# Block-diagonal full-array products and identities on VectorE in the inversion of a delta-rule attention

## The reference

```
k_n = k / (norm(k) + 1e-6);  state = zeros(B, H, 48, 48)
for t in range(768):
    y[t]  = q[t] @ state
    v_old = state^T k_n[t]
    state = state + beta[t] * outer(k_n[t], v[t] - v_old)
x = y as (3072, 384)
# experts: logits = x @ w_gate; e = argmax; out = gate * sigmoid(x @ w_output_gate)[e] * relu(x @ w1[e]) @ w2[e]
# last:    max(x @ w1, x @ w2, x @ w3) @ w_out
```

## Time and profile before

| | us |
|---|---|
| runs (median of 3) | 1111.56 (1108.06 to 1112.52) |
| the profiled execution's own time | 1108.98 |
| its span | 1107.3 |
| TensorE busy | 1026.3 |
| VectorE busy | 509.7 |
| ScalarE busy | 366.9 |
| GpSimd busy | 335.4 |

### The profile page before, as it was taken

The page is one execution under the profiler, slowest core; times in us unless marked ns, Lnnn a source line. Parts: engine busy times, 40 slices in busy tenths (PEclk is TensorE's granted clock), DMA queues, the critical chain, the costliest instruction groups (busy, mean ns, idle before and its releaser), DMA issues. The chain is left out here.

```text
span 1107.3 us, 30948 instructions
## 1 busy us (share of the span) xinstructions
PE 1026.3 (93%) x13260; PEld 895.4 (81%) x13260; DVE 509.7 (46%) x1085; ACT 366.9 (33%) x731; POOL 335.4 (30%) x251
## 2 busy tenths in 40 slices
PE   4898999999999999849999999999599999999998
PEld 3787888887888778737999999998488888888888
DVE  5575665666666655435444444433332323233221
ACT  1455544554555455412222222221121222122111
POOL 3444253435233422115352555525310001000000
PEclk9999998999999999958999999999699999999999
DMA  9212112121212111044344444223201010100000
GB/s 313 110 34 65 55 53 60 55 72 41 72 58 70 41 44 34 9 151 162 102 155 165 171 165 171 86 86 114 71 22 39 19 44 14 48 16 22 15 15 29
DMA packets 58056, 84.90 MB, mean 77 GB/s; under 512 B 28880, under 2 KB 52816, under 8 KB 55376
## 3 DMA queue, kind: packets, MB, share of 16 engines
q1 hardware_dynamic: 52272, 46.94, 13.5%
q0 software_dynamic: 5664, 36.18, 9.6%
HBM read 61.67 MB, written 21.43 MB: 75 GB/s over the span
## 5 line engine op out<-in xcount | busy, mean ns | idle before, releaser
L1081 PE MATMUL hb<-early,last_h 128*128 128x512 f32 x648 | 208.0, 402 | 1.2 <-DVE early L1213 1.2
L1081 PEld LDWEIGHTS hb<-early,last_h 128*128 128x128 f32 x648 | 121.7, 191 | 29.4 <-DVE early L1213 1.6
L1081 PE MATMUL hb<-early,last_l 128*128 128x512 f32 x324 | 129.3, 399 | 0.0
L1219 DVE TENSOR_TENSOR m<-hb,m 128x512 f32<-128x512 f32 x36 | 24.9, 692 | 132.3 <-PE hb L1081 132.3
L329 PEld LDWEIGHTS bank<-t,n_hi 64*64 64x64 f16 x2688 | 65.7, 111 | 23.6 <-issue 7.9
L540 DVE TENSOR_TENSOR p<-bank,cf 128x512 f16<-128x512 f32 x96 | 66.1, 689 | 32.2 <-PE bank L329 31.8
L329 PE MATMUL bank<-t,n_hi 64*64 64x64 f16 x2688 | 72.7, 195 | 4.9 <-issue 4.2
L1081 PE MATMUL ob<-wo_h,early 128*128 128x384 f32 x288 | 75.1, 339 | 0.0
L1081 PEld LDWEIGHTS hb<-early,last_l 128*128 128x128 f32 x324 | 61.6, 190 | 15.0
L1003 POOL TENSOR_TENSOR late<-w_raw,late 128x3072 fp32r<-128x3072 f32 x8 | 54.5, 6812 | 57.6 <-DVE late L943 57.3
L1114 POOL DMA_INDIRECT rows<-y_sorted,idx x24 | 23.0, 959 | 159.1 <-DVE scaled L1209 155.8
(11 more groups left out here) (163 smaller groups left out, 2194.7 us busy)
## 6 DMA issues: line engine op xcount, KB each, us to landing
w_raw<-w POOLq DMA_DIRECT2D x14, 1536.0 KB, 7.6
kq_t<-qh SPq DMA_DIRECT2D x24, 256.0 KB, 3.3
y_sorted<-y_sb SPq DMA_DIRECT2D x31, 192.0 KB, 1.9
x_in<-x_sorted SPq DMA_DIRECT2D x29, 192.0 KB, 2.8
k_raw<-kt_in SPq DMA_DIRECT2D x24, 192.0 KB, 3.2
v_in<-vh SPq DMA_DIRECT2D x24, 192.0 KB, 3.6
k_own<-kh SPq DMA_DIRECT2D x24, 192.0 KB, 3.4
out<-o_sb SPq DMA_DIRECT2D x24, 192.0 KB, 1.8
```

Source lines behind the costliest of these rows:

```text
L1081: ins = pe.matmul(out, a[x], b[y], start=first and i == 0, stop=last and i == 2, skip_group_check=True)
L1219: dve.tensor_tensor(m1[f % 2][:], h_bank[f % 2][1][:, :], m0[f % 2][:], ALU.max).then_inc(m1_out, 1)
```

## The change

In the inversion of the attention stage:
- The identities of the three jacobi rounds and of the residual are no longer added by PE. VectorE adds them when it reads PSUM: instead of a multiplication by the block mask it now does an addition of the identity, and in the residual (which moves from ScalarE to VectorE) of twice the identity.
- Since the mask is no longer applied to the result, N is masked beforehand: GpSimd computes n_base, N times the mask of 4x4 blocks, in slot 2, and jacobi waits for it in place of n_hi.
- "inv" is one product, residual plus twice the identity times the transpose, so that the product of t16 and the identity goes.
- Five groups (prod at four levels and N times t16 in the residual) use n_both: for each head a 128x128 block-diagonal matrix with both halves' N, so that 8 full-array matmuls with 64 columns take the place of 16. ScalarE fills n_both with two copies behind n_hi; its zeros are written once at the start. Minus t16 in the residual is one full-array matmul of 512 columns.
- Five parts of the norm move one slot ahead, GpSimd's kn waits for beta_k from the second step on, and in "lg" VectorE reads the logits from PSUM instead of waiting for its own copy.

```diff
-    ch[:, CH_REP:CH_REP + U * C] = np.tile(row == col, (1, U))
+    ch[:, CH_REP:CH_REP + C] = row == col
...
-    NORM = {1: [0], 2: [1], 3: [2, 10], 5: [3], 6: [4], 7: [5], 8: [6, 13], 9: [7, 8, 9], 14: [11], 15: [12]}
+    NORM = {1: [0], 2: [1], 3: [2, 10], 4: [3], 5: [4], 6: [5], 7: [6], 8: [7, 8, 9, 13], 14: [11], 15: [12]}
...
+        def both_heads(lhs, rhs, out, first=False):
+            for u in range(U):
+                ins = pe.matmul(out[:, C * u:C * u + C], lhs[:, u].rearrange("q h c -> q (h c)"), rhs(u), start=first and u == 0,
+                                stop=True, skip_group_check=True)
+            return ins
+        def whole(lhs, rhs, out, first):
+            return pe.matmul(out[:, :], lhs, rhs, start=first, stop=True, skip_group_check=True)
...
             elif what == "jacobi":
-                    pe.wait_ge(n_hi_ready[st], k + 1)
+                    pe.wait_ge(n_base_ready[st], k + 1)
...
-                diagonal(ident16, ident_rep, pb, True)
-                each_head(n, eye if lv == 0 else t, pb).then_inc(jacobi_done[st], 1)
+                each_head(nb, eye if lv == 0 else t, pb, first=True).then_inc(jacobi_done[st], 1)
...
             elif what == "prod":
...
-                each_head(n, t, pb, first=True).then_inc(prod_done[st], 1)
+                both_heads(n_both[st], lambda u: t16[st][:, u, :], pb, first=True).then_inc(prod_done[st], 1)
...
             elif what == "resid":
-                diagonal(ident16, ident_rep, pb, True)
-                diagonal(neg16, flat(t16[st]), pb, False)
-                each_head(n, t, pb)
+                whole(neg16, flat(t16[st]), pb, True)
+                both_heads(n_both[st], lambda u: t16[st][:, u, :], pb)
                 each_head(nl, t, pb).then_inc(resid_done[st], 1)
             elif what == "inv":
...
-                each_head(t, eye, ttb, first=True)
                 pe.wait_ge(resid_out[st], k + 1)
-                each_head(pr, tt, ttb).then_inc(inv_done[st], 1)
+                each_head(pr, tt, ttb, first=True).then_inc(inv_done[st], 1)
... (ScalarE)
                 act.copy(n_hi[st][:], n_kb_a[par][st][:, :, 0, :]).then_inc(n_hi_ready[st], 1)
+                for hh, s in enumerate(half):
+                    ins = act.copy(n_both[st][s, :, hh, :], n_kb_a[par][st][s, :, 0, :])
+                ins.then_inc(n_both_ready[st], 1)
...
-            elif what == "resid":
-                act.copy(p16[st][:], pb).then_inc(resid_out[st], 1)
... (VectorE)
-                dve.tensor_tensor(t16[st][:], pb, mask_of(None), ALU.mult).then_inc(jacobi_out[st], 1)
+                dve.tensor_tensor(t16[st][:], pb, of_heads(CF_EYE), ALU.add).then_inc(jacobi_out[st], 1)
+            elif what == "resid":
+                dve.wait_ge(resid_done[st], k + 1)
+                dve.tensor_tensor(p16[st][:], pb, of_heads(CF_TWO), ALU.add).then_inc(resid_out[st], 1)
...
-                dve.tensor_copy(logits[:, to, :], yb[st][:, X:X + 2 * E]).then_inc(logit_out[st], 1)
-                dve.wait_ge(logit_out[st], k + 1)
-                dve.tensor_reduce(best[:, st:st + 1], logits[:, to, 0:E], AX.X, ALU.max).then_inc(routed[st], 1)
+                dve.tensor_reduce(best[:, st:st + 1], yb[st][:, X:X + E], AX.X, ALU.max).then_inc(routed[st], 1)
+                dve.tensor_copy(logits[:, to, :], yb[st][:, X:X + 2 * E])
... (GpSimd)
             if what == "kn":
-                pool.wait_ge(inv_norm, k + 1)
+                if k >= 1:
+                    pool.wait_ge(beta_k_ready, k + 1)
+                else:
+                    pool.wait_ge(inv_norm, 1)
...
+            elif what == "split":
+                pool.wait_ge(gram_out[st], 2 * k + 2)
+                pool.tensor_tensor(n_base[st][:], n_kb_a[par][st][:, :, 0, :], of_heads(CF_BASE), ALU.mult).then_inc(n_base_ready[st], 1)
```

More of the change, by code:

```diff
@@ L40 @@
 CF_BASE = CF_LV + (LEVELS - 2) * C
-CF_IOTA = CF_BASE + C
+CF_EYE = CF_BASE + C
+CF_TWO = CF_EYE + C
+CF_IOTA = CF_TWO + C
 CF_STEP = CF_IOTA + E
@@ L49 @@
 CH_REP = CH_NEG + P
-CH_TRI = CH_REP + U * C
+CH_TRI = CH_REP + C
 CH_ONE = CH_TRI + P
@@ L69, in constants @@
         cf[:, CF_LV + (lv - 2) * C:CF_LV + (lv - 1) * C] = below & ((col >> lv) == (row >> lv) - 1)
-    cf[:, CF_BASE:CF_BASE + C] = (row >> 2 == col >> 2) & (row >= col)
+    cf[:, CF_BASE:CF_BASE + C] = row >> 2 == col >> 2
+    cf[:, CF_EYE:CF_EYE + C] = row == col
+    cf[:, CF_TWO:CF_TWO + C] = 2.0 * (row == col)
     cf[:, CF_IOTA:CF_IOTA + E] = E - np.arange(E)
@@ L129, in attention_and_router @@
     n_hi = single("n_hi", [P, U, C], F16)
+    n_both = single("n_both", [P, U, 2, C], F16)
     n_lo = single("n_lo", [P, U, C], F16)
+    n_base = single("n_base", [P, U, C], F16)
     t16 = single("t16", [P, U, C], F16)
@@ L177, in attention_and_router @@
     n_lo_ready = pair_of("n_lo_ready")
+    n_both_ready = pair_of("n_both_ready")
+    n_base_ready = pair_of("n_base_ready")
     kb_ready = pair_of("kb_ready")
@@ L217, in attention_and_router @@
     neg16 = ch[:, CH_NEG:CH_NEG + P]
-    ident_rep = ch[:, CH_REP:CH_REP + U * C]
+    eye16 = ch[:, CH_REP:CH_REP + C]
     tri16 = ch[:, CH_TRI:CH_TRI + P]
@@ L342, in eye @@
         def eye(s, u):
-            return ident_rep[s, 0:C]
+            return eye16[s, :]
         def inv(k, par, st, what, lv):
             tb, ttb, pb = bank[st]
-            n, nl, t, tt, pr = (lambda s, u, x=x[st]: x[s, u, :] for x in (n_hi, n_lo, t16, tt16, p16))
+            nl, nb, t, tt, pr = (lambda s, u, x=x[st]: x[s, u, :] for x in (n_lo, n_base, t16, tt16, p16))
             if what == "kt":
@@ L517, in norm, with clear @@
                 act.activation(nrm[:, 1], nrm[:, 0], ACT.Sqrt).then_inc(rooted, 1)
+                if k == 0:
+                    clear(n_both[1])
+        def clear(x):
+            for hh, s in enumerate(half):
+                act.copy(x[s, :, 1 - hh, :], zeros[s, 0:C].unsqueeze(1).broadcast_to((C, U, C)))
         act.wait_ge(zeros_ready, 1)
         act.activation(root_of_zero[:], zeros[:, 0:1], ACT.Sqrt)
+        clear(n_both[0])
         act.wait_ge(blank, 1)
@@ L561, in chain @@
                 to = 2 * k + st
-                dve.tensor_copy(logits[:, to, :], yb[st][:, X:X + 2 * E]).then_inc(logit_out[st], 1)
-                dve.wait_ge(logit_out[st], k + 1)
-                dve.tensor_reduce(best[:, st:st + 1], logits[:, to, 0:E], AX.X, ALU.max).then_inc(routed[st], 1)
+                dve.tensor_reduce(best[:, st:st + 1], yb[st][:, X:X + E], AX.X, ALU.max).then_inc(routed[st], 1)
+                dve.tensor_copy(logits[:, to, :], yb[st][:, X:X + 2 * E])
                 dve.wait_ge(routed[st], 5 * k + 1)
-                dve.scalar_tensor_tensor(out=score[st][:], in0=logits[:, to, 0:E], scalar=best[:, st:st + 1],
+                dve.scalar_tensor_tensor(out=score[st][:], in0=yb[st][:, X:X + E], scalar=best[:, st:st + 1],
                                          in1=cf[:, CF_IOTA:CF_IOTA + E], op0=ALU.is_equal, op1=ALU.mult).then_inc(routed[st], 1)
```

12 lines of the change are left out of this document (5 added, 7 removed).

## The result

| | before | after |
|---|---|---|
| runs, median | 1109.81 (4 runs, 1105.80 to 1112.52) | 1127.59 (4 runs, 1122.01 to 1144.68) |
| profiled execution, span | 1107.3 | 1120.3 |

The ratio is 1.0152, 95% interval 1.0108 to 1.0195. The medians in this document are over all runs of a kernel, while the ratios leave out its slow runs, those over 1.5% above its fastest (here the one at 1144.68). The forecast was 1105 with a range up to 1118: wrong in sign, and outside the range. The profiled execution, at 1122.01 us, is the fastest of the four.

The account below looks back on a forecast made before the run. PE, busy 93% of the span, bounds the kernel. Per attention step -0.9 + 1.0 - 0.3 - 0.1 = -0.3 us, -4 over 12 steps, -2 for fewer gaps: -6, so 1105 us; 8-in-10 range 1088 to 1118.

Parts of the forecast that it names:

- GpSimd's new wait: GpSimd ahead of n_base: holds back 5 us of work whose users come four slots later or more; no cost.
- ScalarE's copies: Slots 2 to 3: two n_both copies, 0.5 us each, behind n_hi delay t; stretch to level-4 product 2.83 to 3.8 us.
- a full-array group: PE's prod and residual groups: 8 full-array matmuls of 64 columns take 0.24 us, loads hidden, no change.
- the 0.1 us for a change of array form: PE: each switch between quarter-array and full-array work costs 0.1 us.
- Rival C: PE's full-array loads aren't hidden: 0.063 us a matmul, 0.50 a group; +18 us, near 1130; chance 0.14.
- Jacobi's wait in slot 12: PE's wait for n_hi ahead of stage 1's first jacobi product, 0.5 us with latency, goes.
- the wait ahead of ks in slot 10: PE's 0.73 us idle before ks, behind VectorE's beta_k products and place, stays; stretch only 0.1 us earlier.
- The count of changes of array form: PE, full step: 36 changes before, 43 afterwards; 7 x 0.1 = 0.7 us a step more.
- PE's own sum: PE per step, were it never to wait: 2 x 1.12 - 0.7 = 1.55 us less.
- the full-array products: Prod and residual groups through n_both: 0.24 us a group as before, so no saving in themselves.
- fewer gaps: Attention stage: unexplained 1.25 us gaps, once a step, 15 us, fall with 16% fewer matmuls; 2 us less.
- The clock: PE's clock dropping more often than now was named as one thing that would make the prediction wrong; no size.

Follow-up runs that it names:

- experiment 5: Kernel after with n_both copies in ScalarE's slot 4, the norm clamp as TENSOR_REDUCE and the choice as SCALAR_TENSOR_TENSOR: 1107.17 us, ratio 0.9958 to before.
- 2: Kernel after with n_base made by VectorE instead of GpSimd: 1119.03 us, ratio 1.0078 to before.
- experiment 4: Kernel after with n_base on VectorE and the n_both copies in ScalarE's slot 4: 1088.93 us, ratio 0.9809 to before.
- 8: Kernel after without n_both and its copies (64x64 products again), n_base on GpSimd: 1137.46 us, ratio 1.0244 to before.
- 6: Kernel after without n_both and its copies (64x64 products again), n_base on VectorE: 1104.58 us, ratio 0.9958 to before.
- experiment 3: Kernel after with the n_both copies in ScalarE's slot 4, behind t, instead of slot 2: 1134.01 us, ratio 1.0217 to before.
- 1: Kernel after with the norm parts back in their old slots: 1128.20 us, ratio 1.0188 to before.
- 11: Kernel after with n_base on VectorE, n_both copies in slot 4 and norm parts in their old slots: 1086.89 us, ratio 0.9805 to before.
- experiment 10: Kernel after with n_base on VectorE and six filler products ahead of slot 3's wait: 1116.14 us, ratio 1.0040 to before.
- the fillers: Products with unread results ahead of PE's waits: on kernel after (slot 3 and "turn") 1134.29 us; with n_base on VectorE (slot 3 only) 1116.14 us.

## Why the prediction was wrong

**The step that failed** is the cost of GpSimd's new wait: "Behind the new wait on GpSimd stand kb, the send, kn and the next mask: 5 us of work whose users come four slots later or more", and the prediction gave that no cost. I asked who waits for the results of the delayed work, and nobody does. I didn't ask what the delayed work does to the other engines while it runs. It runs without a pause in the slots of the norm clamp and of the choice, and holds these up through two or three instructions: the clamp goes from 165 to 1,886 ns in the median, the choice from 231 to up to 1,959. PE's waits behind the two, 3.7 and 1.4 us before, are 13.4 and 7.3. Shown by experiment 5 (the form alone: -26.8 us), by 2 and 4, and by 8 against 6 (the engine of n_base alone: 32.9 us).

The Trainium skill (SBUF — State Buffer, Who interferes with whom) has this rule: VectorE and GpSimd share a pair of SBUF ports, which is an exclusive lock; a tensor_scalar can take it in its two-port modes, an instruction with two SBUF inputs contends with GpSimd's reads, and tensor_reduce never contends. The traces agree on all three, behind the same queue: the clamp as a tensor_scalar takes 3,150 ns in the median (experiment 3) and as a tensor_reduce 178 at most (experiment 5), and the choice with two SBUF inputs takes up to 2,394. It was the rule that spoke against this change, and the prediction didn't weigh it. One could have priced it from the kernel before: 5 us of GpSimd work moved onto two small VectorE operations, each of which can be stretched by the two or three GpSimd instructions running then (1.9, 1.2). And the kernel before shows the effect itself, in a row that the prediction used: its four beta_k products, with both operands in SBUF, take 1.25 us while GpSimd's kn runs beside them.
```profile
360.05 0.83 POOL L664 TENSOR_TENSOR kn<-k_raw,nrm 128x384 f32<-128x384 f32 x1 [11.31 <-DVE nrm L607]
```
In the kernel after, where kn waits for beta_k, the same four take 0.69 us (below). I took the 1.25 us as given and didn't ask what they were made of.

**ScalarE's copies** were seen rightly and sized a little too small: 1.26 us, not 1.0, so slot 3 takes 4.11, not 3.8. That is 0.3 x 12 = 4 us more. PE's idle time there is 14.7 us in 11 steps, 1.3 each, where 1 was forecast.

**Right**: a full-array group takes 0.24 us. Timeline after, PE, a group and the start of the next:
```profile
252.72 0.41 PE L342 MATMUL bank<-t,n_both 128*128 128x64 f16 x8
...
252.96 0.53 PE L462 MATMUL chain<-cf,y_tile 128*128 128x128 f32 x3
```
Where a 64x64 group follows, the next start comes after 0.32 to 0.34 us, so the 0.1 us for a change of array form holds too. Rival C is out, and so is the 0.43 us that I worked out from the Trainium skill (TensorE: Matmul & The Clock Gate, Back-to-back issue gap): the measurement decides. Jacobi's wait in slot 12 is gone. n_base is in time in slot 3, with 0.1 of margin where 0.2 was forecast.

**Wrong, small**: the wait ahead of ks in slot 10 was to stay. Timeline after:
```profile
340.22 0.69 DVE L644 TENSOR_TENSOR beta_k<-nrm,beta 64x8 f32<-64x8 f32 x4
...
340.60 0.66 PE L369 MATMUL bank<-cf,kn 128*128 128x128 f32 x4
341.21 1.10 PE L435 MATMUL chain<-state,kq_t 128*128 128x96 f32 x8
```
No idle time stands there any more (0.73 before). The larger part is that kn now waits for beta_k, so the four products take 0.56 us less; with the norm parts back (experiments 1 and 11) they still take 0.69, and 0.17 us of idle time is left in most steps. The shift of the norm took away only that rest, which is why it brought nothing measurable. What the wait of kn is worth by itself no run shows.

The count of changes of array form was off as well. By the program's order, with gram counted as 64x64 work and "z" as full-array work, a full step has 32 before and 36 after: 4 more, not 7. PE's own sum would be 1.84 us a step, not 1.55; the forecast, bound by other engines, hardly hung on it.

**Wrong, hidden by the loss**: the full-array products were to be worth nothing by themselves, plus 2 us for fewer gaps. In the version without the waits they are worth 15.7 (experiments 4 and 6). The idea that gaps without a visible wait go with the number of matmuls had the right sign and was far too small. Why these gaps come is open: they stand at issue, with no wait in the program.

**The clock** was named as what would make the prediction wrong. In the stage it is 0.95, before 0.98, and the stage's slices of the page have more eights. Over repeated runs of one and the same kernel, 1 us more at the lower level of 1.2 GHz (twice the missing share of the clock, times the time) goes with 0.3 us more time for the kernel before (50 runs) and 0.43 for the kernel of experiment 10 (10 runs). After has 109 us of it (2 x (1 - 0.9515) x 1127.6), before 58. At 0.3 to 0.43 the difference would be worth 15 to 22 us of the 17.8 lost. In the versions it goes with the waits (median over the runs 0.9715 in experiment 4, 0.9435 in experiment 3), but going together isn't a cause, and the fillers didn't settle it. How the loss splits can be seen in part. The kernel after and that of experiment 4 have the same number of instructions; from the first to the last copy of t_inv:
```profile
40.90:484.00 443.10, 394.58 (x8260) 345.04 (x8261) 284.93 (x687) 234.06 (x486) 186.23 (x185) 0.95 0.17 49
```
```profile
41.40:450.90 409.50, 382.24 (x8259) 335.16 (x8260) 281.92 (x709) 232.99 (x485) 157.66 (x159) 0.98 0.18 53
```
Of the 33.6 us between them 21.3 are idle time of PE, and 12.3 are more busy time for as many matmuls, at the lower clock. So between these two executions somewhat under two thirds are waits, and the rest goes with the clock.

## What to carry to other kernels

Before an instruction with a wait goes into a queue, ask not only who uses what stands behind it, but beside which instructions of other engines that work will now run: GpSimd's work moved onto VectorE's small SBUF-to-SBUF operations makes each of them last through two or three of GpSimd's instructions. When two new waits cover for each other, undoing one shows little (8.6 us less and 6.4 more here, against 38.7 less for both); undo both, then one at a time from there. And a change that slows a kernel may hold a gain: here 2% came out once n_base stood on VectorE and the copies a slot or two later.

## What was not expected of the hardware

- A VectorE instruction of 16 numbers per partition takes 0.165 us or up to 3.6 us, depending on what GpSimd does beside it. It didn't get its turn between the mask, n_lo and the piece of the weight split, which follow each other without a pause: in the timeline above it waited through all three. Ahead of kb, which follows as closely, it did. What makes the difference wasn't tested.
- The form decides: beside GpSimd's work, TENSOR_SCALAR from SBUF to SBUF up to 3,633 ns, SCALAR_TENSOR_TENSOR with two SBUF operands up to 2,394, TENSOR_REDUCE 178.
- Full-array f16 matmuls with 64 columns and a fresh 128x128 load each follow each other at 0.03 us (0.24 for 8), as fast as pairs of 64x64 ones. Between a full-array group and a 64x64 one it takes 0.1 us more.
- With 9,373 recorded matmuls in 430 us PE stood 23.0 us ahead of 64x64 groups with no wait in the program, with 8,520 it stood 8.0 (24.7 and 14.3 ahead of all groups, from the first to the last inversion). Why is open.
